# Which engine makes the low parts of the input pieces: GpSimd in place of VectorE for 171 of 243

## The chip, the cores and the metric

One NeuronCore of one Trainium2 chip runs the kernel. The metric is the device time of one execution in microseconds (us), smaller is better. Engines are named as in the profile: PE is TensorE, DVE is VectorE, ACT is ScalarE, POOL is GpSimd, SP is SyncE, which here only starts DMAs.

## The reference

Two attentions in a row for each of 8 batches and 8 heads (576 positions, head size 64, 32 packed queries), then two feed-forward layers on the 4608 tokens. All is float32; names are shortened here.

```python
def sm_attn(qq, kk, vv):
    s = scale * np.matmul(qq, kk.transpose(0, 1, 3, 2))
    s = s - np.max(s, axis=-1, keepdims=True)
    a = np.exp(s)
    a = a / (np.sum(a, axis=-1, keepdims=True) + 1e-09)
    return np.matmul(a, vv)
p_packed = sm_attn(p, k, v)
out = sm_attn(q, p_packed, p_packed)
...
h = x @ w_in                       # 512 -> 2048
g = np.maximum(h, 0.0) + alpha * np.minimum(h, 0.0)
y = g @ w_out                      # 2048 -> 512
...
g = y @ w_gate                     # 512 -> 1536
silu = g * (1.0 / (1.0 + np.exp(-g)))
val = y @ w_val
out = silu * val @ w_out2
```

## The kernel before

Every product is made from split operands. A float32 operand x is kept as a high part, x rounded to the type that TensorE multiplies fast (fp32r), and a low part, x minus the high part. `product` (L778 to L780) then issues three matmuls: high by high, low by high, high by low. The high part of an operand is a copy on ScalarE (L1119), the low part a subtraction on VectorE (`subtract`, L1441).

The inputs come in 243 pieces, each up to 128 x 576: 28 of keys ("k"), 35 of values ("v"), 28 of queries ("q"), 64 of w_in ("w"), 16 of w_out ("o"), and 72 for the second layer: 36 of its weights ("g") and 36 sums of them ("s"). SP loads a piece into a ring of four raw buffers (`load`, L605), once the low part of the piece four before it is made, since that frees the buffer. ScalarE makes the high part and VectorE the low part, both in `split`, into a second ring of four (`piece_`, tile name `piece`; w_out has its own place, tile name `w`). A slot of that ring is free once TensorE has used the piece, or, for "g" and "s", once a DMA that GpSimd starts has written it to DRAM (`w_scratch`, L760 and L762, `d_scratch`, L757). The semaphore `piece_high` counts high parts, `piece_split` low parts.

Each engine runs its own program in its own order. One list, `PLAN`, sets all of them. It has 256 slots, one for each of 16 chunks of 288 tokens by 16 tiles of w_in's columns. In a slot TensorE makes one tile of h (6 matmuls, names `h<-attn,mixed`), and adds the tile of two slots before to y (12 matmuls, `acc<-g,w`, L986 and L990). Between them ScalarE takes the negative part of h (L1276), VectorE combines it with alpha into gF (L1633), ScalarE makes g's high part (L1119), VectorE its low part (L1441, `g<-floats,g`). Each of these goes some slots ahead of its use. The attention of the following batches, the products with w_in that go ahead (`mix`, tiles `side` and `mixed`), the pieces ("split" entries, one to three slots before their use) and the keeping of the second layer's weights ("keep" entries) are put into the slots as further entries. Attention on VectorE is a chain: L1483 (maximum), L1578 (transposes), L1584, L1586 (subtract maximum), L1591 to L1595, L1601 (normalise), L1605 (transpose).

A piece's low part is waited for in five places: by SP for the raw ring, by TensorE (`piece_ready`), by GpSimd for a "keep", by the sums of second-layer weights on VectorE, and by ScalarE before the buffer of these sums is used again. GpSimd's own program has a few memsets, `clear` entries (a memset of packF), the keeps and the stores of y (L767).

After the slots the second layer runs from the kept weights in five runs; no input piece is made there.

Of the kernel before, what the change touches and what calls it, by code (L numbers as in the profile page):

```python
# [284 lines left out]

PIECES = [e[1] for e in PLAN if e[0] == "split"]
PIECE_NO = {p: n for n, p in enumerate(PIECES)}
RAWS = [p for p in PIECES if p[0] != "s"]
RAW_NO = {p: n for n, p in enumerate(RAWS)}
AHEAD = RAW_NO["g", EARLY_KEEPS - 1, 0]  # L290
# [28 lines left out]
def build(nc, kT, vS, qT, pT, w_in, w_out, alpha, w_gate, w_val, w_down, out):  # L319
# [3 lines left out]
    with ExitStack() as ctx:  # L323
# [43 lines left out]
        def f(at, n):  # L367
            return F[:, at:at + n]
# [107 lines left out]
        ident_zeroed, ident_ready = sem("ident_zeroed"), sem("ident_ready")  # L476
        both_zeroed, both0_zeroed, packF_zeroed = sem("both_zeroed"), sem("both0_zeroed"), sem("packF_zeroed")
        nalpha_ready = sem("nalpha_ready")
        piece_high, piece_split, piece_left = sem("piece_high"), sem("piece_split"), sem("piece_left")
        p_high, p_split = sem("p_high"), sem("p_split")  # L480
        scores1_done, max1_ready, exp1_done, rec_ready, den1_step = (
            sem("scores1_done"), sem("max1_ready"), sem("exp1_done"), sem("rec_ready"), sem("den1_step"))
# [78 lines left out]
            return (f(4224, 1024) if j < EARLY_KEEPS else late_sums[:, :])  # L561


        def unsplit(p):

            return weight_sums(p[1])[:, 512 * p[2]:512 * p[2] + 512] if p[0] == "s" else raw(p)
# [17 lines left out]
        def _(sp):  # L584
            once = Once(sp)

            def load(p):
                if RAW_NO[p] >= RING:
                    once.wait_ge(piece_split, PIECE_NO[RAWS[RAW_NO[p] - RING]] + 1)
                dst = raw(p)  # L590
                if p[0] == "k":
                    src = kT[p[1], p[2], :, :]
                elif p[0] == "q":
                    dst = dst.rearrange("p (i n) -> p i n", i=2)
                    src = qT[p[1], 2 * p[3]:2 * p[3] + 2, :, p[2] * CH:(p[2] + 1) * CH].rearrange("i p n -> p i n")
                elif p[0] == "v":
                    dst = dst[rows(p[2]), :]
                    src = vS[p[1], p[2] * P:min((p[2] + 1) * P, SEQ), :]
                elif p[0] == "w":
                    src = w_in[p[3] * P:(p[3] + 1) * P, p[2] * CW:(p[2] + 1) * CW]  # L600
                elif p[0] == "o":
                    src = w_out[p[1]]
                elif p[0] == "g":
                    src = (w_gate, w_val)[p[2]][p[1]] if p[1] < NT2 else w_down[2 * (p[1] - NT2) + p[2]]
                sp.dma_start(dst, src).then_inc(raw_landed[raw_slot(p)], 16)  # L605
# [29 lines left out]
            def load_y(r, ks=range(KD)):  # L635
                if r:
                    once.wait_ge(block_step, steps_to(r - 1, T_ORDER[-1]))
                else:
                    once.wait_ge(attn_split, NCH)
                    once.wait_ge(attnF_ready, NCH - 1)  # L640
                    once.wait_ge(piece_split, PIECE_NO["s", EARLY_KEEPS - 1, 1] + 1)
                once.wait_ge(y_stored, 16 * min(NCH, -(-(START_OF[r] + 2 * HALF[r]) // CH)))
                for k in ks:
                    sp.dma_start(yraw[:, k, :, 0:HALF[r]],
                                 yT[k, :, START_OF[r]:START_OF[r] + 2 * HALF[r]].rearrange("p (c n) -> p c n", c=2)
                                 ).then_inc(y_landed, 16)
# [86 lines left out]
        @block.gpsimd  # L733
        def _(pool):
            once = Once(pool)
            pool.dma_start(alphas, alpha).then_inc(alpha_landed, 16)
            nc.gpsimd.memset(ident, 0.0).then_inc(ident_zeroed, 1)
            once.wait_ge(ident_zeroed, 1)
# [4 lines left out]
            once.wait_ge(t1_done, 2)  # L743
            nc.gpsimd.memset(f(4224, 512), 0.0).then_inc(both0_zeroed, 1)
            for e in PLAN:
                if e[0] == "clear":
                    if e[1] == 1:
                        once.wait_ge(pT_done, 2)
                    else:
                        once.wait_ge(packT_done, e[1] - 1)  # L750
                    nc.gpsimd.memset(f(7104, 512), 0.0).then_inc(packF_zeroed, 1)
                elif e[0] == "keep":
                    p = pieces_of(e)[0]
                    once.wait_ge(piece_split, PIECE_NO[p] + 1)
                    if e[1] >= NT2:
                        for s in range(1 if e[2] == 0 else 2):
                            pool.dma_start(dS[e[1] - NT2, e[2], s], piece(p)[:, :, 256 * s:256 * s + 256].bitcast(F32)  # L757
                                           ).then_inc(kept[e[2]], 16)
                    elif e[2] == 1:
                        pool.dma_start(wS[e[1], :, 1, :, 256:512], piece(p)[:, :, 256:512].bitcast(F32)).then_inc(kept[e[2]], 16)  # L760
                    else:
                        pool.dma_start(wS[e[1], :, e[2], :, :], piece(p).bitcast(F32)).then_inc(kept[e[2]], 16)  # L762
                elif e[0] == "ycopy":
                    c = e[1]
                    once.wait_ge(y_copied_act, 2 * c + 2)
                    once.wait_ge(y_copied_dve, 2 * c + 2)
                    pool.dma_start(yT[:, :, c * CH:(c + 1) * CH].rearrange("m p n -> p m n"), ystage  # L767
                                   ).then_inc(y_stored, 16)
# [5 lines left out]
        def _(pe):  # L774
# [20 lines left out]
                once.wait_ge(mix_split, mixes_before(e))  # L795

            def piece_ready(p):
                once.wait_ge(piece_split, PIECE_NO[p] + 1)

            def scores1_0(half):  # L800
                once.wait_ge(p0_ready, 1)
# [313 lines left out]
        def _(act):  # L1115
# [87 lines left out]
            def exp1(e):  # L1203
                _, b, half = e
                once.wait_ge(max1_ready, NTH[e] + 1)
                if b == 1:
                    once.wait_ge(mix_done, 2 * KD)
                    once.wait_ge(rec1_ready, 2)
                else:
                    once.wait_ge(turned, ST * (b - 1))  # L1210
                    once.wait_ge(rec_ready, 2 * (b - 1))
                sums = before(e, "sums") // 2
                if sums:
                    once.wait_ge(piece_split, PIECE_NO["s", sums - 1, 1] + 1)
                nc.scalar.activation(s1[:, half, :].rearrange("p (c n) -> p c n", c=2), scores,
                                     ACT.Exp, bias=nmax1[:, half:half + 1], accum_out=sum1[:, half:half + 1]
                                     ).then_inc(exp1_done, 1)
# [129 lines left out]
            def copy_lead(r):  # L1347

                once.wait_ge(tile_done, NTILES * r + TILE_NO["B11", PAIRS - 1] + 1)
                if r == 0:  # L1350
                    once.wait_ge(y_stored, 16 * NCH)
                    once.wait_ge(piece_split, len(PIECES))
                once.wait_ge(out_stored[11], 16 * r)
                copy(lead[:, :, 0:HALF[r]], acc[:, 0:2, 0:HALF[r]]).then_inc(lead_copied, 1)

# [81 lines left out]
        def _(dve):  # L1437
# [2 lines left out]
            def subtract(dst, x, high):  # L1440
                return nc.vector.tensor_tensor(dst, x, high.bitcast(F32), ALU.subtract)  # L1441

            def split(p):
                n = PIECE_NO[p]
                k, c = piece_rows(p), piece_columns(p)
                once.wait_ge(piece_high, n + 1)
                subtract(piece(p)[k, 1, c], unsplit(p)[k, c], piece(p)[k, 0, c]).then_inc(piece_split, 1)

            def sums(e):

# [7 lines left out]
                if half == 0:  # L1458
# [1 line left out]
                    if j >= EARLY_KEEPS:  # L1460
                        once.wait_ge(packed_done, B - 1)
                    if j:
                        once.wait_ge(piece_split, PIECE_NO["s", j - 1, 1] + 1)
                    for p in (g_no, v_no):
                        once.wait_ge(raw_landed[raw_slot(p)], landed(p))
                    nc.vector.tensor_tensor(s1_, a21, a22, ALU.add).then_inc(sums_step, 1)
# [302 lines left out]
            for e in PLAN:  # L1769
# [15 lines left out]
                    attn_0(e[1])  # L1785
                elif e[0] == "alpha":
                    alpha_1()
                elif e[0] == "split":
                    split(e[1])
                elif e[0] == "split_p":  # L1790
                    split_p(e[1])
                elif e[0] == "max1":
# [117 lines left out]
```

## Time and profile before

| | |
|---|---|
| median of three runs | 1597.93 us (1597.17 to 1599.99) |
| the profiled execution | 1597.42 us, of which the span is 1595.2 us |
| PE busy | 98% |
| DVE busy | 72% |
| ACT busy | 46% |
| POOL busy | 5% |

The span is the stretch from the first to the last instruction that the profiler saw; all times of rows count from its start. A row of a timeline is one instruction, or several of one kind in a run; in brackets stands how long the engine was idle before it and which engine's instruction ended that. The first layer fills the span to about 800 us, the second the rest. Matmuls of 288 columns follow each other at about 0.13 us and are shown with their latency of 0.29 us, so that small gaps between them can't be seen as idle time.

### The profile page before, as it was taken

The numbers are of one execution on the slowest core, as the hardware profiler recorded it, in microseconds if no ns is written. First come the engines' busy times: TensorE is split into PE (matmuls) and PEld (weight loads), VectorE is DVE, ScalarE is ACT, GpSimd is POOL, SyncE is SP. The second block draws the span as 40 slices with busy tenths as digits, with TensorE's granted clock in tenths as the row PEclk, the third lists the DMA queues.
The fourth block names the chain that finished last, engine by engine and source line by source line (L and its number), as shares of the span: only waits on it lengthen the run. The fifth ranks groups of instructions, "written<-read, shape, count | busy, mean of one in ns | idle before, by whom it ended". The sixth has DMA issues, their size and how long they took to land.

```text
span 1595.2 us, 24866 instructions
## 1 busy us (share of the span) xinstructions
PE 1562.7 (98%) x9330; PEld 1436.2 (90%) x9330; DVE 1148.5 (72%) x2010; ACT 728.5 (46%) x1475; POOL 76.3 (5%) x123
## 2 busy tenths in 40 slices
PE   8999999999999999999999999999999999999999
PEld 5899988989999999999988888888888889999998
DVE  5777679868698687987865577556765685667666
ACT  4565568555685656745532144223412252233223
POOL 0000000100001000014300000000000000000000
PEclk9999999999999999999999999999999999999999
DMA  7343225523345233338665665766667667877856
GB/s 269 111 126 115 79 73 161 166 87 120 115 123 178 65 131 121 98 147 293 213 219 192 238 212 178 245 235 217 192 213 237 215 200 248 300 271 238 290 203 218
DMA packets 132502, 293.15 MB, mean 184 GB/s; under 512 B 13456, under 2 KB 41120, under 8 KB 132384
## 3 DMA queue, kind: packets, MB, share of 16 engines
q1 hardware_dynamic: 120544, 249.08, 49.0%
q0 software_dynamic: 11840, 42.48, 7.0%
q8 instruction: 75, 1.23, 0.3%
q14 instruction: 43, 0.35, 0.1%
HBM read 239.61 MB, written 51.90 MB: 183 GB/s over the span
## 4 chain that ended last, share of the span: by engine, by line
PE 80%; DVE 13%; ACT 3%; issue 2%; DMA 1%; ACTq 0%; DVEq 0%
PE acc L986 9%; PE side L778 9%; PE side L779 9%; PE side L780 9%; PE h L778 8%; PE h L780 8%; PE h L779 8%; PE acc L990 5%; PE acc L778 5%; PE acc L780 4%; PE acc L779 4%; DVE piece L1441 3%; DVE mixed L1441 2%; DVE floats L1633 2%; DVE g L1441 1%
## 5 line engine op out<-in xcount | busy, mean ns | idle before, releaser
L986 PE MATMUL acc<-g,w 128*128 128x288 f32 x1792 | 272.4, 294 | 0.0
L986 PEld LDWEIGHTS acc<-g,w 128*128 128x128 f32 x1792 | 249.0, 188 | 0.0
L1119 ACT ACTIVATE g<-floats 128x288 fp32r<-128x288 f32 x256 | 113.8, 444 | 223.3 <-DVE floats L1633 152.5
L1441 DVE TENSOR_TENSOR g<-floats,g 128x288 fp32r<-128x288 f32 x256 | 115.2, 450 | 68.0 <-ACT g L1119 66.5
L1323 ACT ACTIVATE rows_b<-side 128x512 f32<-128x512 f32 (+1 forms) x60 | 33.4, 557 | 285.6 <-PE side L780 285.6
L1441 DVE TENSOR_TENSOR piece<-floats,piece 128x512 fp32r<-128x512 f32 (+3 forms) x217 | 143.5, 682 | 25.2 <-ACT piece L1119 22.5
L778 PE MATMUL h<-attn,mixed 128*128 128x288 f32 x512 | 157.8, 308 | 3.5 <-DVE floats L1633 2.1
L1633 DVE SCALAR_TENSOR_TENSOR floats<-floats,h 128x288 f32<-128x288 f32 x256 | 130.4, 509 | 39.9 <-ACT floats L1276 38.3
L990 PE MATMUL acc<-g,w 128*128 128x288 f32 x896 | 156.2, 296 | 0.2 <-DVE g L1441 0.2
L780 PE MATMUL h<-attn,mixed 128*128 128x288 f32 x512 | 151.3, 295 | 0.0
L779 PE MATMUL h<-attn,mixed 128*128 128x288 f32 x512 | 151.2, 295 | 0.0
L990 PEld LDWEIGHTS acc<-g,w 128*128 128x128 f32 x896 | 131.2, 188 | 0.5 <-DVE g L1441 0.5
L1119 ACT ACTIVATE piece<-floats 128x512 fp32r<-128x512 f32 (+3 forms) x217 | 128.2, 616 | 3.5 <-PE side L780 2.1
L1276 ACT ACTIVATE floats<-h 128x288 f32<-128x288 f32 x256 | 102.7, 401 | 39.5 <-PE h L780 38.0
L778 PEld LDWEIGHTS h<-attn,mixed 128*128 128x128 f32 x512 | 96.3, 188 | 10.9 <-DVE floats L1633 3.1
L1329 ACT ACTIVATE rows_a<-rows_a 128x512 f32<-128x512 f32 (+1 forms) x60 | 35.4, 590 | 143.6 <-DVE rows_a L1696 143.6
L779 PEld LDWEIGHTS h<-attn,mixed 128*128 128x128 f32 x512 | 96.4, 188 | 3.3 <-issue 1.0
L780 PEld LDWEIGHTS h<-attn,mixed 128*128 128x128 f32 x512 | 96.3, 188 | 0.0
L1681 DVE TENSOR_TENSOR rows_b<-side,rows_a 128x512 f32<-128x512 f32 (+1 forms) x60 | 38.3, 638 | 71.6 <-PE side L780 71.3
L1671 DVE TENSOR_TENSOR rows_a<-side,rows_a 128x512 f32<-128x512 f32 (+1 forms) x60 | 38.3, 638 | 64.2 <-PE side L780 64.2
L1119 ACT ACTIVATE tiles_b<-u_a 128x512 fp32r<-128x512 f32 (+3 forms) x80 | 61.7, 778 | 47.2 <-PE acc L780 24.6
L1441 DVE TENSOR_TENSOR mixed<-side,mixed 64x512 fp32r<-64x512 f32 (+1 forms) x112 | 76.9, 687 | 5.1 <-ACT mixed L1119 3.8
(284 smaller groups left out, 3810.5 us busy)
## 6 DMA issues: line engine op xcount, KB each, us to landing
ring<-w_scratch SPq DMA_DIRECT2D x90, 512.0 KB, 4.4
wring<-d_scratch SPq DMA_DIRECT2D x168, 256.0 KB, 2.9
ring_c<-w_scratch SPq DMA_DIRECT2D x60, 512.0 KB, 4.1
w_scratch<-piece POOLq DMA_DIRECT2D x36, 512.0 KB, 4.0
floats<-w_in SPq DMA_DIRECT2D x64, 256.0 KB, 3.2
ring_b<-w_scratch SPq DMA_DIRECT2D x30, 512.0 KB, 4.8
d_scratch<-piece POOLq DMA_DIRECT2D x42, 256.0 KB, 3.8
ring<-d_scratch SPq DMA_DIRECT2D x42, 256.0 KB, 3.0
```

Source lines behind the costliest of these rows:

```text
L778: pe.matmul(dst, w[0], x[0], start=start, stop=False, **kw)
L779: pe.matmul(dst, w[1], x[0], start=False, stop=False, **kw)
L780: return pe.matmul(dst, w[0], x[1], start=False, stop=stop, **kw)
L986: pe.matmul(acc[:, m, 0:CH], w2[:, j, x, m * P:(m + 1) * P], g[:, s % 2, 0, :], start=False, stop=False)
L990: mm = pe.matmul(acc[:, m, 0:CH], w2[:, j, 0, m * P:(m + 1) * P], g[:, s % 2, 1, :], start=False, stop=False)
L1119: return nc.scalar.activation(dst, src, ACT.Copy, **kw)
L1276: nc.scalar.activation(gF[:, s % 2, :], hb[s % 2][:, 0:CH], ACT.Relu, scale=-1.0).then_inc(neg_done, 1)
L1329: nc.scalar.activation(first_two[:, 0:h], first_two[:, 0:h], ACT.Silu).then_inc(silu2_ready, 1)
L1441: return nc.vector.tensor_tensor(dst, x, high.bitcast(F32), ALU.subtract)
L1633: nc.vector.scalar_tensor_tensor(out=gF[:, s % 2, :], in0=gF[:, s % 2, :], scalar=alphas[:, j:j + 1], in1=hb[s % 2][:, 0:CH], op0=ALU.mult ...
L1671: nc.vector.tensor_tensor(first_two[:, 0:h], set_banks[1][:, 0:h], first_term[:, 0:h], ALU.add).then_inc(two_ready, 1)
L1681: nc.vector.tensor_tensor(first_three[:, 0:h], set_banks[1][:, 0:h], first_term[:, 0:h], ALU.add).then_inc(three_ready, 1)
```

## The change

Low parts of "k", "v", "q", "w" and "o" pieces, 171 of them, are made by GpSimd (`input_low`, `BY_POOL`), at the place of the "split" entry in GpSimd's program. The 72 of "g" and "s" stay on VectorE (`weight_low`, `BY_DVE`). GpSimd has a semaphore of its own, `input_split`; `low_of` tells each waiting engine which semaphore and value a piece has. High parts stay on ScalarE, and `PLAN` is the same. The memset of a `clear` waits for the low parts that stand ahead of it, and each low part for the one before it.

```diff
+BY_POOL = [p for p in PIECES if p[0] in "kvqwo"]
+BY_DVE = [p for p in PIECES if p[0] in "gs"]
...
+        def low_of(p):
+
+            return (input_split, BY_POOL.index(p) + 1) if p in BY_POOL else (piece_split, BY_DVE.index(p) + 1)
...
+            def input_low(p):
+                k, c = piece_rows(p), piece_columns(p)
+                once.wait_ge(input_split, BY_POOL.index(p))
+                once.wait_ge(both0_zeroed, 1)
+                once.wait_ge(packF_zeroed, before(("split", p), "clear") + 1)
+                once.wait_ge(piece_high, PIECE_NO[p] + 1)
+                nc.gpsimd.tensor_tensor(piece(p)[k, 1, c], unsplit(p)[k, c], piece(p)[k, 0, c].bitcast(F32), ALU.subtract
+                                        ).then_inc(input_split, 1)
...
             for e in PLAN:
-                if e[0] == "clear":
+                if e[0] == "split" and e[1] in BY_POOL:
+                    input_low(e[1])
+                elif e[0] == "clear":
...
+                    once.wait_ge(input_split, sum(p in BY_POOL for p in PIECES[:before(e, "split")]))
...
-            def split(p):
-                n = PIECE_NO[p]
-                k, c = piece_rows(p), piece_columns(p)
-                once.wait_ge(piece_high, n + 1)
-                subtract(piece(p)[k, 1, c], unsplit(p)[k, c], piece(p)[k, 0, c]).then_inc(piece_split, 1)
+            def weight_low(p):
+                c = piece_columns(p)
+                once.wait_ge(piece_high, PIECE_NO[p] + 1)
+                subtract(piece(p)[:, 1, c], unsplit(p)[:, c], piece(p)[:, 0, c]).then_inc(piece_split, 1)
```

Three places of the instruction order follow. The lines of the changed kernel are some 20 higher: L1441 is L1461 there, L1601 is L1620, L1633 is L1652.

The first is VectorE between the end of an attention chain and the next slots, at 497 to 502 us of the trace. `piece` of 576 columns is a query. Before:

```order
L1441 TENSOR_TENSOR g<-floats,g 128x288
L1441 TENSOR_TENSOR piece<-floats,piece 128x576
L1633 SCALAR_TENSOR_TENSOR floats<-floats,h 128x288
L1601 TENSOR_TENSOR floats<-floats 128x576
L1605 STREAM_TRANSPOSE floats<-floats 128x576
L1441 TENSOR_TENSOR g<-floats,g 128x288
L1441 TENSOR_TENSOR piece<-floats,piece 128x576
```

After:

```order
L1461 TENSOR_TENSOR g<-floats,g 128x288
L1652 SCALAR_TENSOR_TENSOR floats<-floats,h 128x288
L1620 TENSOR_TENSOR floats<-floats 128x576
L1624 STREAM_TRANSPOSE floats<-floats 128x576
L1461 TENSOR_TENSOR g<-floats,g 128x288
L1652 SCALAR_TENSOR_TENSOR floats<-floats,h 128x288
```

The two queries' low parts are gone from the row; all else keeps its order.

The second is GpSimd from 457 to 491 us, the end of the w_in pieces of batch 4 and the fifth set of second-layer weights. L762 and L760 before (L782 and L780 after) are keeps. Before:

```order
37 L767 DMA y_scratch<-floats 128x4x288 [waits y_copied_dve,y_copied_act]
38 L762 DMA w_scratch<-piece 128x1024 [waits piece_split]
39 L760 DMA w_scratch<-piece 128x2x256 [waits piece_split]
```

After:

```order
94 L787 DMA y_scratch<-floats 128x4x288 [waits y_copied_dve,y_copied_act]
95 L750 TENSOR_TENSOR piece<-floats,piece 128x512 [waits piece_high,input_split] x5
96 L750 TENSOR_TENSOR piece<-floats,piece 128x576 [waits piece_high,input_split] x2
97 L782 DMA w_scratch<-piece 128x1024 [waits piece_split]
98 L780 DMA w_scratch<-piece 128x2x256 [waits piece_split]
```

The keeps now stand behind two queries' low parts, whose high parts ScalarE makes later than the kept piece.

The third is VectorE at 566 to 572 us, a pair of keys that TensorE uses at once (`x2`), and pieces of the second layer around it. Before:

```order
L1578 STREAM_TRANSPOSE floats<-side 128x288 x2
L1441 TENSOR_TENSOR g<-floats,g 128x288
L1441 TENSOR_TENSOR piece<-floats,piece 128x576 x2
L1441 TENSOR_TENSOR piece<-floats,piece 128x512
L1633 SCALAR_TENSOR_TENSOR floats<-floats,h 128x288
```

After:

```order
L1597 STREAM_TRANSPOSE floats<-side 128x288 x2
L1461 TENSOR_TENSOR g<-floats,g 128x288
L1461 TENSOR_TENSOR piece<-floats,piece 128x512
L1652 SCALAR_TENSOR_TENSOR floats<-floats,h 128x288
```

The pair stands on GpSimd instead, between the keeps of the two 512-column pieces around it.

## Rows read from the trace of the kernel before

**Rows 1.** The page, busy time and share of the span of each engine.

```profile
PE 1562.7 (98%) x9330; PEld 1436.2 (90%) x9330; DVE 1148.5 (72%) x2010; ACT 728.5 (46%) x1475; POOL 76.3 (5%) x123
```

**Rows 2.** Table by stretch; columns: stretch, length, busy time by engine, clock, DMA.

```profile
30.00:700.00 670.00, 649.00 (x4640) 623.32 (x4639) 530.56 (x1057) 415.53 (x941) 36.63 (x59) 1.00 0.37 118
```

**Rows 3.** Groups by shape, VectorE: line, names, shapes, count, busy us, mean ns, idle before.

```profile
L1441 DVE TENSOR_TENSOR g<-floats,g 128x288 fp32r<-128x288 f32 x256 | 115.2, 450 | 68.0 <-ACT g L1119 66.5
L1441 DVE TENSOR_TENSOR piece<-floats,piece 128x512 fp32r<-128x512 f32 x136 | 91.8, 687 | 15.9 <-ACT piece L1119 13.9
...
L1441 DVE TENSOR_TENSOR piece<-floats,piece 128x576 fp32r<-128x576 f32 x56 | 40.2, 753 | 7.7 <-ACT piece L1119 7.3
...
L1441 DVE TENSOR_TENSOR w<-floats,w 128x512 fp32r<-128x512 f32 x16 | 11.0, 687 | 2.3 <-ACT w L1119 2.1
```

**Rows 4.** Groups by shape, GpSimd.

```profile
L751 POOL MEMSET floats<- 128x512 f32 x7 | 3.8, 542 | 6.0 <-PE h L830 6.0
...
L739 POOL TENSOR_SCALAR_AFFINE_SELECT floats<-floats 128x128 f32<-128x128 f32 x1 | 0.3, 282 | 0.2 <-POOL floats L737 0.2
...
L1904 POOL MEMSET const-float32-0.0<- 128x1 f32 x1 | 0.1, 99 | 0.2 <-issue 0.2
```

**Rows 5.** Timeline of PE, matmuls that waited: start, length, instruction, idle before.

```profile
76.93 0.39 PE L778 MATMUL side<-piece,pp 128*128 128x256 f32 x1 [1.41 <-DVE pp L1441]
...
158.91 0.39 PE L778 MATMUL side<-piece,pp 128*128 128x256 f32 x1 [0.68 <-DVE pp L1441]
...
209.40 0.38 PE L778 MATMUL side<-piece,pp 128*128 128x256 f32 x1 [0.69 <-DVE pp L1441]
...
230.87 0.53 PE L778 MATMUL side<-piece,both 128*128 128x512 f32 x1 [1.17 <-DVE both L1441]
...
248.03 0.50 PE L778 MATMUL side<-piece,both 128*128 128x512 f32 x1 [1.37 <-DVE mixed L1441]
...
286.70 0.40 PE L778 MATMUL h<-attn,mixed 128*128 128x288 f32 x1 [0.48 <-DVE floats L1633]
...
304.98 0.37 PE L778 MATMUL acc<-g,w 128*128 128x288 f32 x1 [0.85 <-DVE g L1441]
...
377.55 0.37 PE L778 MATMUL side<-piece,pp 128*128 128x288 f32 x1 [0.77 <-issue]
...
501.07 0.37 PE L778 MATMUL acc<-g,w 128*128 128x288 f32 x1 [0.84 <-DVE g L1441]
```

**Rows 6.** Timelines of DVE and PE's weight loads around three places with keys.

```profile
325.14 1.43 DVE L1441 TENSOR_TENSOR piece<-floats,piece 128x576 fp32r<-128x576 f32 x2 [1.11 <-ACT piece L1119]
...
326.62 0.19 PEld L778 LDWEIGHTS side<-piece,pp 128*128 128x128 f32 x1 [0.17 <-DVE piece L1441]
...
385.44 0.76 DVE L1441 TENSOR_TENSOR piece<-floats,piece 128x576 fp32r<-128x576 f32 x1 [1.11 <-ACT piece L1119]
...
386.63 0.19 PEld L778 LDWEIGHTS side<-piece,pp 128*128 128x128 f32 x1
...
569.42 2.03 DVE L1441 TENSOR_TENSOR piece<-floats,piece 128x576 fp32r<-128x576 f32 x3
...
570.90 0.19 PEld L778 LDWEIGHTS side<-piece,pp 128*128 128x128 f32 x1 [0.17 <-DVE piece L1441]
```

**Rows 7.** Timeline of DVE ahead of the wait at 501.07.

```profile
497.94 0.75 DVE L1441 TENSOR_TENSOR piece<-floats,piece 128x576 fp32r<-128x576 f32 x1
...
499.02 0.75 DVE L1601 TENSOR_TENSOR floats<-floats 128x576 f32<-128x576 f32 x1
```

**Rows 8.** Timelines of POOL and ACT, and the page's DMA issues (count, KB, us to landing).

```profile
474.97 0.53 POOL L762 DMA_DIRECT2D w_scratch<-piece  x1 [16.43 <-DVE piece L1441]
...
478.15 1.24 ACT L1119 ACTIVATE piece<-floats 128x576 fp32r<-128x576 f32 x2
...
485.43 0.61 ACT L1119 ACTIVATE piece<-floats 128x512 fp32r<-128x512 f32 x1
...
w_scratch<-piece POOLq DMA_DIRECT2D x36, 512.0 KB, 4.0
```

More of the change, by code:

```diff
@@ L478, in build @@
         nalpha_ready = sem("nalpha_ready")
-        piece_high, piece_split, piece_left = sem("piece_high"), sem("piece_split"), sem("piece_left")
+        piece_high, piece_left = sem("piece_high"), sem("piece_left")
+        piece_split, input_split = sem("piece_split"), sem("input_split")
         p_high, p_split = sem("p_high"), sem("p_split")
@@ L588, in load @@
                 if RAW_NO[p] >= RING:
-                    once.wait_ge(piece_split, PIECE_NO[RAWS[RAW_NO[p] - RING]] + 1)
+                    once.wait_ge(*low_of(RAWS[RAW_NO[p] - RING]))
                 dst = raw(p)
@@ L640, in load_y @@
                     once.wait_ge(attnF_ready, NCH - 1)
-                    once.wait_ge(piece_split, PIECE_NO["s", EARLY_KEEPS - 1, 1] + 1)
+                    once.wait_ge(*low_of(("s", EARLY_KEEPS - 1, 1)))
                 once.wait_ge(y_stored, 16 * min(NCH, -(-(START_OF[r] + 2 * HALF[r]) // CH)))
@@ L753, in _ @@
                     p = pieces_of(e)[0]
-                    once.wait_ge(piece_split, PIECE_NO[p] + 1)
+                    once.wait_ge(*low_of(p))
                     if e[1] >= NT2:
@@ L797, in piece_ready @@
             def piece_ready(p):
-                once.wait_ge(piece_split, PIECE_NO[p] + 1)
+                once.wait_ge(*low_of(p))
             def scores1_0(half):
@@ L1213, in exp1 @@
                 if sums:
-                    once.wait_ge(piece_split, PIECE_NO["s", sums - 1, 1] + 1)
+                    once.wait_ge(*low_of(("s", sums - 1, 1)))
                 nc.scalar.activation(s1[:, half, :].rearrange("p (c n) -> p c n", c=2), scores,
@@ L1351, in copy_lead @@
                     once.wait_ge(y_stored, 16 * NCH)
-                    once.wait_ge(piece_split, len(PIECES))
+                    once.wait_ge(piece_split, len(BY_DVE))
                 once.wait_ge(out_stored[11], 16 * r)
@@ L1462, in sums @@
                     if j:
-                        once.wait_ge(piece_split, PIECE_NO["s", j - 1, 1] + 1)
+                        once.wait_ge(*low_of(("s", j - 1, 1)))
                     for p in (g_no, v_no):
@@ L1787, in _ @@
                     alpha_1()
-                elif e[0] == "split":
-                    split(e[1])
+                elif e[0] == "split" and e[1] in BY_DVE:
+                    weight_low(e[1])
                 elif e[0] == "split_p":
```

## Prediction

> **What bounds the kernel now.** I read the page's busy shares first. TensorE is busy 98% of the span [rows 1], at a granted clock of 1.00 in the stretch that matters [rows 2], so a change elsewhere can only give back TensorE's idle time or add to it. Then the table by stretch: the moved subtractions stand between 30 and 700 us, and there TensorE is busy 649.0 of 670 us. So at most 21.0 us can be given back, while VectorE is busy 530.6 us and GpSimd 36.6 us [rows 2]. VectorE is the fuller of the two, but an average says little. What counts is which wait ends last in front of a matmul. The timeline of TensorE names it: nine of its larger waits in the stretch end on VectorE, or on a queue behind it, with a low part of an input piece shortly ahead in VectorE's row [rows 5]. And a few matmuls start the moment a low part of a key is made [rows 6]. These two lists are the two sides of the sum.
>
> **What is removed.** 171 of 243 low parts leave VectorE: 64 of w_in, 35 of values, 28 of keys, 28 of queries, 16 of w_out. 99 pieces of 512 columns at 687 ns are 68.0 us, 56 of 576 columns at 753 ns are 42.2 us, 16 of w_out at 687 ns are 11.0 us: 121.2 us in all [rows 3]. Nearly all of it lay beside matmuls. What was on the path is the part in front of TensorE's waits. At 497.94 a query's low part runs 0.75 us on VectorE; behind it come L1633, L1601, L1605 and the low part of g, and a matmul has waited 0.84 us for the last of these at 501.07 [rows 5, 7]. The order's first place shows the query's step gone from between them. In the same way I credit each wait with the moved low parts directly ahead of it, never more than the wait itself: 0.69 at 76.93, 0.68 at 158.91, 0.69 at 209.40, 0.69 at 230.87, 0.69 at 248.03, 0.48 at 286.70, 0.75 at 304.98, 0.77 at 377.55 (two keys ahead), 0.75 at 501.07. The sum is 6.2 us [rows 5]. That is the upper end. The lower end is zero: what is late next is the link of the chain that VectorE does not shorten (TensorE's turn, ScalarE's copy), and the subtractions that leave may cost VectorE something beside GpSimd (below). Waits whose VectorE row had been idle, or had only pieces of the second layer ahead, get no credit. Between the ends I take the middle, 3.1 us, since neither end has a row that is nearer.
>
> **What is added.** 171 subtractions on GpSimd. Its trace shows no instruction with two inputs, so the price is bounded. Below: the memset of 128x512, which only writes, took 542 ns, and TENSOR_SCALAR_AFFINE_SELECT, which reads one input, took 282 ns for 128 columns, against 99 ns for one column: 1.44 ns a column, which makes 0.84 us for 512 columns and 0.93 us for 576. Above: the same with the second input read after the first, 1.58 us and 1.76 us [rows 4]. A subtraction has two inputs, so it should lie over the one-input line; I take the middle, 1.2 us for 512 and 1.35 us for 576. The Trainium skill (GPSIMD Engine Reference, section 3.1) has 4497 ns for a tensor_tensor of 2048 columns. By that page an estimate would be 1.1 and 1.25 us, and the sum below would be about 0.6 us smaller. No run here shows it. In all it is some 205 us of GpSimd's 670, so throughput holds.
>
> A low part now comes 0.5 to 0.6 us later by itself, and the second of a pair 1.2 us later, since both queue on one slower engine. That costs nothing where the matmul comes several us later, as it does for most pieces; the cover is the lead that the plan gives. It costs where there is no lead. The second key of a pair is at 326.62: VectorE began the pair at 325.14, and the weights were loaded 0.05 us after its end [rows 6]. GpSimd starts about 0.17 us later than VectorE did (L739 there waited 0.2 us for a semaphore of its own engine [rows 4]; VectorE follows ScalarE at once), and then makes 2 x 1.35 us: 325.14 + 0.17 + 2.70 + 0.05 = 328.06, so 1.44 us later than 326.62. The pair at 569.42 with its matmul at 570.90 gives 1.43 us, and a third pair, at 579, repeats the pattern: 4.3 us. The single key at 385.44 gives 385.44 + 0.17 + 1.35 + 0.05 = 387.01 against 386.63, 0.4 us [rows 6]. Sum 4.7 us. With the low price (0.93 us, no later start) it is 3 x 0.4 = 1.2 us; with the high one (1.76 us) 3 x 2.3 + 0.8 = 7.6 us. The pieces of w_in with as little lead cost nothing: on VectorE they stood behind low parts of mixed and g, which GpSimd does not have.
>
> **What is moved past what.** GpSimd also issues the DMAs that keep the second layer's weights and store y. A DMA that stands behind a low part now waits for that piece's high part. At the order's second place the DMA of the first piece of a set, issued at 474.97, comes behind both queries [rows 8]. ScalarE makes both high parts from 478.15 on in 1.24 us, the first by about 478.8, so the DMA goes at about 478.8 + 0.2 + 2.7 = 481.7. With 4.0 us to landing that is 485.7, and ScalarE wants the slot at 485.43 [rows 8]: 0.3 us, hidden by the lead of its copies. Where landing takes longer it is the third rival. SP's loads of the input wait for the low part too, and go 0.5 to 1.2 us later; I cost them at nothing, since ScalarE's copies of pieces hardly waited for a load, and name the sign of the contrary below. The w_out pieces and the clears of packF are covered by several us of lead. After 700 us the order is unchanged, so nothing moves there.
>
> **The sum.** 4.7 - 3.1 = +1.6 us on a profiled execution of 1597.42 us (span 1595.2 and 2.2 around it), which stands 0.5 us under the median of the runs, 1597.93. I add it to the median: 1599.5.
>
> **The rivals.**
> First, faster. A low part takes about 0.93 us and VectorE gets all of its time back: +1.2 - 6.2, and the small waits among the 21.0 us give another 1: -6.0, so 1591.9. For it: VectorE is busy 79% of the stretch. Against it: GpSimd's one-input row already gives 0.93, and several of the listed waits are chains from a matmul over ScalarE back to TensorE.
>
> Second, slower, by one mechanism: a GpSimd subtraction and a VectorE instruction with both inputs in SBUF hold each other up. The trace of before cannot show it, since GpSimd there only writes beside VectorE. If one waits for the other's end, VectorE's low part of g (0.45 us, 256 times [rows 3]) or L1601 (0.75 us, [rows 7]) stands up to 1.35 us behind a GpSimd step where its own low part took 0.75. Nothing is then given back, each pair of keys is parted by one VectorE instruction of 0.45 us (3 x 0.45 = 1.4 us), and slots with little lead lose about 1 us: 4.7 + 1.4 + 1.0 = +7.1, so 1605.0. It decides as soon as both engines cannot read at once. The Trainium skill (SBUF — State Buffer, "Who interferes with whom") states just this rule: a VectorE instruction with two SBUF inputs and a GpSimd instruction that reads SBUF exclude each other for a whole instruction. By that rule the time is 1605.0; L1633 and the subtractions from PSUM, with one SBUF input, would be free of it.
>
> Third, late refills: DMAs that keep weights land late, ScalarE's next copy into the slot waits, and with it the high part of g. Four places at 1 us each beyond the forecast: 1603. Against it: other keeps have 7 us or more from issue to reuse.
>
> That the change does not do what it says is ruled out by the order: 171 subtractions stand on GpSimd.
>
> **How the numbers follow.** Forecast 1599.5, chance 0.45, its own range 1596 to 1602. Faster rival 0.24, mutual hold-up 0.23, late refills 0.08. Leaving out about 0.1 at either end gives 1591.5 to 1606. A measurement can tell about 0.2%, 3.2 us, from no change. Faster by that (under 1594.7): 0.20, all from the first rival. Slower (over 1601.1): 0.07 of the forecast, 0.21 of the hold-up, 0.05 of the refills, 0.33. Within: 0.47.
>
> **What would show it.** Right: GpSimd's new group of subtractions has a mean near 1.2 and 1.35 us; VectorE's group of g keeps 450 ns and L1601 0.75 us; the second keys near 327, 571 and 580 us follow waits of over 1 us for GpSimd; the wait at 501.07 is down to about 0.1. Wrong: VectorE's two-input instructions grow or start late with nothing ahead of them while L1633 keeps its length (the hold-up); the new group has a mean under 1 us (faster); ScalarE's copies wait for w_scratch or a load (refills).

## The result and the profile after

The changed kernel takes 1614.55 us (median, 1613.89 to 1616.02). Measured beside it, the kernel before takes 1598.41 us. The ratio is 1.0102, 95% interval 1.0084 to 1.0119: slower by about 16 us, outside the predicted range of 1591.5 to 1606. The profiled execution took 1615.05 us, with a span of 1612.9 us against 1595.2.

The page, busy time and share of the span of each engine; and, from its chain that ended last, the shares by engine:

```profile
PE 1567.3 (97%) x9330; PEld 1439.7 (89%) x9330; DVE 1107.0 (69%) x1839; ACT 731.0 (45%) x1475; POOL 310.6 (19%) x294
...
PE 78%; DVE 15%; ACT 3%; issue 2%; DMA 1%; POOL 1%; SPq 0%; ACTq 0%; DVEq 0%; POOLq 0%
```

Beside [rows 1], VectorE lost 171 instructions, which the prediction put at 121.2 us of work, and its busy time fell by 41.5 us only. TensorE does the same 9330 matmuls, yet is busy 4.6 us longer and idle 13.1 us longer; together these are the 17.7 us by which the span grew. The next views say why. First VectorE and GpSimd by shape (line, names, shapes, count, busy us, mean ns, idle before):

```profile
L1461 DVE TENSOR_TENSOR g<-floats,g 128x288 fp32r<-128x288 f32 x256 | 166.0, 648 | 78.6 <-ACT g L1139 77.1
L1652 DVE SCALAR_TENSOR_TENSOR floats<-floats,h 128x288 f32<-128x288 f32 x256 | 130.3, 509 | 105.0 <-ACT floats L1296 103.7
L1461 DVE TENSOR_TENSOR mixed<-side,mixed 64x512 fp32r<-64x512 f32 x96 | 66.0, 687 | 7.5 <-ACT mixed L1139 6.3
L1461 DVE TENSOR_TENSOR piece<-floats,piece 128x512 fp32r<-128x512 f32 x44 | 34.3, 781 | 8.1 <-ACT piece L1139 7.2
...
L1620 DVE TENSOR_TENSOR floats<-floats 128x576 f32<-128x576 f32 x15 | 15.9, 1061 | 0.0
...
L1605 DVE TENSOR_TENSOR floats<-floats 128x576 f32<-128x576 f32 x15 | 13.9, 928 | 0.5
```

```profile
L750 POOL TENSOR_TENSOR piece<-floats,piece 128x512 fp32r<-128x512 f32 x92 | 121.1, 1316 | 158.1 <-ACT piece L1139 156.0
L750 POOL TENSOR_TENSOR piece<-floats,piece 128x576 fp32r<-128x576 f32 x56 | 83.0, 1482 | 102.2 <-ACT piece L1139 100.2
...
L750 POOL TENSOR_TENSOR w<-floats,w 128x512 fp32r<-128x512 f32 x16 | 21.3, 1329 | 28.3 <-ACT w L1139 27.9
```

The low part of g, untouched by the change, went from a mean of 450 ns [rows 3] to 648 ns. The pieces of 512 columns that stayed went from 687 to 781 ns, L1620 (L1601 before) from 0.75 us [rows 7] to 1061 ns. All of these read two inputs from SBUF. L1652 and the low part of `mixed` read one operand from PSUM (`h`, `side`); they stand at 509 and 687 ns, and in the zero-filled kernels below, where GpSimd reads nothing, L1652 again has 511 ns. I sorted the 256 low parts of g by whether a GpSimd subtraction was under way: 183 without one have a mean of 0.452 us, 73 with one 1.141 us, the longest 2.06 us. Of the low parts of g that began while a subtraction ran (68), 60 ended 0.31 to 0.33 us after its end and none later than 0.42 us after it, however much of it was still to run. GpSimd is held too: its subtractions of 512 columns took 1.41 us in the mean where a VectorE TENSOR_TENSOR with both inputs in SBUF was under way at their start (24), and 1.29 us where none stood beside them (42); with 576 columns 1.60 us (18) and 1.43 us (15).

What such a meeting looks like stands at the very place for which the prediction expected a wait to shrink to 0.1 us. The timeline of all engines at 509.75 to 514.4 us (start, length, engine, instruction, idle before):

```profile
509.87 1.57 POOL L750 TENSOR_TENSOR piece<-floats,piece 128x576 fp32r<-128x576 f32 x1 [4.16 <-ACT piece L1139]
510.06 0.50 DVE L1652 SCALAR_TENSOR_TENSOR floats<-floats,h 128x288 f32<-128x288 f32 x1
510.48 1.56 DVE L1620 TENSOR_TENSOR floats<-floats 128x576 f32<-128x576 f32 x1
...
512.08 0.78 DVE L1624 STREAM_TRANSPOSE floats<-floats 128x576 f32<-128x576 f32 x1
512.14 1.41 POOL L750 TENSOR_TENSOR piece<-floats,piece 128x576 fp32r<-128x576 f32 x1
512.78 1.09 DVE L1461 TENSOR_TENSOR g<-floats,g 128x288 fp32r<-128x288 f32 x1
...
514.02 0.37 PE L798 MATMUL acc<-g,w 128*128 128x288 f32 x1 [1.79 <-DVE g L1461]
```

L1652 (one SBUF input) keeps its 0.50 us beside the GpSimd step. L1620 starts beside it and ends 0.60 us after its end at 511.44; the low part of g ends at 513.87, 0.32 us after GpSimd's end at 513.55. Here the query's low part, 0.75 us, is gone from VectorE, but L1620 takes 0.81 us more and g 0.68 us more (its length at 500.51 was 0.41 us before), and the matmul, which had waited 0.84 us before [rows 5], now waits 1.79 us.

TensorE's groups of matmuls that wait, by name; the idle time before them is the last column (before the change, in the same order: 3.5, 0.2, 9.0, 2.4 and 3.3 us):

```profile
L798 PE MATMUL h<-attn,mixed 128*128 128x288 f32 x512 | 157.7, 308 | 4.3 <-DVE floats L1652 2.9 <-DVE attn L1461 1.2
L1010 PE MATMUL acc<-g,w 128*128 128x288 f32 x896 | 157.1, 297 | 1.1 <-DVE g L1461 1.1
L798 PE MATMUL side<-piece,pp 128*128 128x288 f32 (+2 forms) x126 | 38.8, 308 | 14.1 <-POOL piece L750 5.9 <-DVE pp L1461 3.6 <-issue 3.0
L798 PE MATMUL acc<-g,w 128*128 128x288 f32 x128 | 38.4, 300 | 7.0 <-DVE g L1461 5.0 <-DVE floats L1667 2.0
L798 PE MATMUL side<-piece,both 128*128 128x512 f32 x64 | 25.9, 405 | 6.2 <-DVE mixed L1461 4.9 <-DVE both L1461 1.0 <-POOL piece L750 0.3
```

They add up to 14.3 us more (all other groups together wait 1.2 us less), in two kinds: matmuls that wait for GpSimd's low part of a piece, and matmuls that wait for VectorE, although VectorE has fewer instructions than before: for its low parts of g and of `mixed`, and for L1667, a copy out of PSUM (2.0 of the 7.0 us). The low part of `mixed` keeps its length, so it comes late by what stands ahead of it. At the longest wait, which ends at 249.79, that is a low part of g of 1.41 us, where before the change it took 0.46 us; from its start to that of the low parts of `mixed` it is 4.05 us instead of 3.71, although a piece's 0.69 us between them is gone.

The third part is the clock. Table by stretch, TensorE alone (stretch, length, busy, granted clock, DMA share, GB/s); before the change the clock is 1.00 in the stretch [rows 2]:

```profile
249.00:251.00 2.00, 1.21 (x7) 1.00 0.39 112
251.00:253.00 2.00, 2.00 (x12) 0.56 0.47 88
253.00:255.00 2.00, 2.00 (x10) 0.58 0.90 331
255.00:257.00 2.00, 2.00 (x16) 1.00 0.65 106
333.00:335.00 2.00, 1.24 (x6) 0.54 0.55 146
335.00:337.00 2.00, 2.00 (x10) 0.50 0.38 120
337.00:339.00 2.00, 2.00 (x11) 0.50 0.00 0
339.00:341.00 2.00, 2.00 (x13) 0.75 0.03 8
341.00:343.00 2.00, 2.00 (x17) 1.00 0.02 4
```

In two places TensorE runs at 1.2 GHz instead of 2.4. The first follows a wait of 2.10 us for the low part of `mixed` that ends at 249.79, the second the waits for the first pair of keys (1.92 us, then 0.76 us). The missing clock shares, 0.44 and 0.42 of 2 us and 0.46, 0.50, 0.50 and 0.25 of 2 us, sum to 5.1 us. That is at most what the half clock costs, since TensorE was also idle in part of it, and it is near the 4.6 us by which its busy time grew. The split is rough: short gaps between matmuls count as busy, and zero_lows below, which never had the half clock, is busy 3.0 us less than the kernel before.

Which wait is followed by the half clock isn't shown. In keys_stay (below) TensorE waits 2.08 us for the same low part of `mixed`, until 249.84, and the clock stays at 1.00. Of the other profiled executions quarters has 17.1 us at half clock, against 10.2 us here; zero_late, keys_zero, only_w, only_q and only_vo have one stretch of 3.4 us each, and the rest none before the end of the span.

### The profile page after: what moved, and what is told of

Read it like the earlier page. It is cut to its first block, busy times and chain, and to the rows that moved or that the text cites. A ratio compares the mean times of both kernels' runs of the same rounds, so it can differ in the third digit from the quotient of the medians.

```text
span 1612.9 us, 25044 instructions
## 1 busy us (share of the span) xinstructions
PE 1567.3 (97%) x9330; PEld 1439.7 (89%) x9330; DVE 1107.0 (69%) x1839; ACT 731.0 (45%) x1475; POOL 310.6 (19%) x294
## 4 chain that ended last, share of the span: by engine, by line
PE 78%; DVE 15%; ACT 3%; issue 2%; DMA 1%; POOL 1%; SPq 0%; ACTq 0%; DVEq 0%; POOLq 0%
PE side L798 9%; PE acc L1006 9%; PE side L800 8%; PE side L799 8%; PE h L798 8%; PE h L800 8%; PE h L799 8%; PE acc L798 4%; PE acc L800 4%; PE acc L799 4%; PE acc L1010 4%; DVE g L1461 3%; DVE mixed L1461 2%; DVE floats L1652 2%; DVE piece L1461 1%
## 5 line engine op out<-in xcount | busy, mean ns | idle before, releaser
L750 POOL TENSOR_TENSOR piece<-floats,piece 128x512 fp32r<-128x512 f32 (+1 forms) x155 | 213.2, 1375 | 275.3 <-ACT piece L1139 271.1
L1461 DVE TENSOR_TENSOR g<-floats,g 128x288 fp32r<-128x288 f32 x256 | 166.0, 648 | 78.6 <-ACT g L1139 77.1
L1652 DVE SCALAR_TENSOR_TENSOR floats<-floats,h 128x288 f32<-128x288 f32 x256 | 130.3, 509 | 105.0 <-ACT floats L1296 103.7
L1010 PE MATMUL acc<-g,w 128*128 128x288 f32 x896 | 157.1, 297 | 1.1 <-DVE g L1461 1.1
L1010 PEld LDWEIGHTS acc<-g,w 128*128 128x128 f32 x896 | 131.9, 189 | 2.0 <-DVE g L1461 2.0
L1461 DVE TENSOR_TENSOR mixed<-side,mixed 64x512 fp32r<-64x512 f32 (+1 forms) x112 | 76.9, 687 | 8.2 <-ACT mixed L1139 7.0
```

Of the source, the lines that this page charges most:

```text
L750: nc.gpsimd.tensor_tensor(piece(p)[k, 1, c], unsplit(p)[k, c], piece(p)[k, 0, c].bitcast(F32), ALU.subtract).then_inc(input_split, 1)
L1010: mm = pe.matmul(acc[:, m, 0:CH], w2[:, j, 0, m * P:(m + 1) * P], g[:, s % 2, 1, :], start=False, stop=False)
L1652: nc.vector.scalar_tensor_tensor(out=gF[:, s % 2, :], in0=gF[:, s % 2, :], scalar=alphas[:, j:j + 1], in1=hb[s % 2][:, 0:CH], op0=ALU.mult ...
```

## The experiments

All ran beside the kernel before, in three rounds. "Low parts" are those that the change moves.

| kernel | median, us | ratio, 95% interval |
|---|---|---|
| zero_lows: zeros by two memsets on GpSimd | 1590.41 | 0.9951 [0.9937, 0.9966] |
| short_lows: nearly all cut to 32 columns | 1588.54 | 0.9939 [0.9924, 0.9954] |
| zero_late: zeros by three memsets | 1597.88 | 1.0000 [0.9990, 1.0009] |
| keys_stay: all but the keys on GpSimd | 1607.48 | 1.0064 [1.0044, 1.0084] |
| only_keys: keys (28) on GpSimd | 1606.12 | 1.0050 [1.0033, 1.0067] |
| keys_zero: keys on GpSimd, as zeros | 1599.28 | 1.0005 [0.9995, 1.0014] |
| only_w: w_in (64) on GpSimd | 1601.89 | 1.0028 [1.0017, 1.0040] |
| only_q: queries (28) on GpSimd | 1599.48 | 1.0018 [1.0009, 1.0028] |
| only_vo: values and w_out (51) | 1598.21 | 1.0006 [0.9996, 1.0016] |
| quarters: four instructions a low part | 1614.07 | 1.0110 [1.0095, 1.0125] |

### GpSimd busy for as long, but reading nothing

The theory by now was the second rival of the prediction, the mutual hold-up. Against it stood that GpSimd's low parts are simply late. zero_lows keeps every semaphore and every place of the changed kernel and takes only the reads away:

```diff
-                nc.gpsimd.tensor_tensor(piece(p)[k, 1, c], unsplit(p)[k, c], piece(p)[k, 0, c].bitcast(F32), ALU.subtract
-                                        ).then_inc(input_split, 1)
+                once.wait_ge(piece_high, PIECE_NO[p] + 1)
+                nc.gpsimd.memset(piece(p)[k, 1, c].bitcast(F32), 0.0).then_inc(zero_step, 1)
+                once.wait_ge(zero_step, BY_POOL.index(p) + 1)
+                nc.gpsimd.memset(piece(p)[k, 1, c].bitcast(F32), 0.0).then_inc(input_split, 1)
```

> GpSimd fills the low part of its 171 pieces with zeros, twice with a wait between, in place of the subtraction (the low by high terms of these pieces drop out of the result). It keeps GpSimd's place, queue and about its length (2 x 0.54 us and a wait of 0.2 us, against 1.3 us alone), but reads nothing. Hold-up of reads: VectorE's two-input groups are back at 0.45 and 0.75 us, the time is 1597 to 1602 us. Late low parts as the cause: it stays at 1610 us or more.

Groups by shape of zero_lows, VectorE and GpSimd:

```profile
L1464 DVE TENSOR_TENSOR g<-floats,g 128x288 fp32r<-128x288 f32 x256 | 115.4, 451 | 81.3 <-ACT g L1142 79.8
L1464 DVE TENSOR_TENSOR piece<-floats,piece 128x512 fp32r<-128x512 f32 x44 | 30.2, 688 | 8.1 <-ACT piece L1142 7.2
...
L1623 DVE TENSOR_TENSOR floats<-floats 128x576 f32<-128x576 f32 x15 | 11.3, 752 | 0.0
```

```profile
L752 POOL MEMSET piece<- 128x512 f32 x92 | 48.5, 527 | 164.2 <-ACT piece L1142 162.2 <-POOL floats L774 0.4
L754 POOL MEMSET piece<- 128x512 f32 x92 | 48.4, 526 | 5.3
L752 POOL MEMSET piece<- 128x576 f32 x56 | 32.5, 580 | 108.3 <-ACT piece L1142 106.9
```

The page of zero_lows, busy time:

```profile
PE 1559.7 (98%) x9330; PEld 1434.6 (90%) x9330; DVE 1045.8 (66%) x1839; ACT 730.9 (46%) x1475; POOL 261.1 (16%) x465
```

1590.41 us: 7.5 us under the kernel before, 24 us under the changed one (ratios 0.9951 and 1.0102). It is also under the 1597 to 1602 us that the expectation gave the hold-up, and far from the 1610 us of lateness. A low part here takes 1.11 us (512 columns) or 1.22 us (576) on GpSimd, 0.21 and 0.26 us less than the subtraction. VectorE's lengths are back at those of before, and it is busy 61.2 us less than in the changed kernel; g alone is 50.6 us of that. Against the kernel before it is busy 102.7 us less, and not 121.2: instructions that follow each other at once overlap in the record (two of 753 ns are a run of 1.43 us in [rows 6]). So the change takes 102.7 us of busy time off VectorE and puts 61.2 us back, which leaves the 41.5 us. VectorE's relief is real and worth what the faster rival gave it; what the change loses beyond lateness is in the reading.

short_lows shortens the subtraction itself: all but the first eight low parts and those of w_out cover 32 columns (274 ns each), so most low parts are left stale.

```diff
+                c = c if p[0] == "o" or RINGED.index(p) < 8 else slice(0, 32)
```

> As the changed kernel, but GpSimd subtracts only 32 columns of a piece, except for w_out and the first eight others (the rest of these low parts is stale). Hold-up of reads: each one is short, VectorE has its 121 us back, 1590 to 1597 us; the gap to 1598.4 is what the relief is worth. Late low parts: the same. If the two semaphores or the order on GpSimd cost the time, it stays near 1610 us.

1588.54 us, just under the expected 1590 to 1597, with g at 477 ns. This is the gain if the low parts cost GpSimd hardly anything, only 1.9 us beyond zero_lows. The low parts are not zeros here, so the gain of zero_lows does not come from TensorE multiplying zeros.

### How much is lateness

zero_late adds a third memset to each low part, in the same way as the second. A low part of zeros then takes 1.69 us (512 columns) or 1.86 us (576), longer than the changed kernel's means of 1.32 and 1.48 us, with no read.

> All 171 moved low parts are filled with zeros by three memsets each in a row on GpSimd, about 1.75 us for 512 columns and 1.85 us for 576, so each is later than the subtraction of the changed kernel (1.32 and 1.48 us), yet nothing of it reads SBUF. The computed result is not the reference's. If the loss is the hold-up alone, this stays near the kernel with two memsets, 1590 to 1596 us, as only the pairs of keys are late by another 1.3 us each. If lateness of the low parts is a real part of the loss, it goes above 1598 us.

1597.88 us, 7.8 us over zero_lows (ratios 1.0000 and 0.9951) by the ratios. It fell between the two expected ranges, 1590 to 1596 for the hold-up alone and over 1598 for lateness as a real part. So lateness has a price: 0.6 us more on each low part takes the whole relief away. TensorE's groups of matmuls with idle before them, in zero_lows and then in zero_late:

```profile
L801 PE MATMUL acc<-g,w 128*128 128x288 f32 x128 | 38.4, 300 | 1.3 <-DVE g L1464 1.1
L801 PE MATMUL side<-piece,pp 128*128 128x288 f32 (+2 forms) x126 | 38.0, 301 | 6.7 <-POOL piece L754 2.8 <-issue 2.1 <-DVE floats L1600 1.5
```

```profile
L803 PE MATMUL acc<-g,w 128*128 128x288 f32 x128 | 38.4, 300 | 1.3 <-DVE g L1466 1.2
L803 PE MATMUL side<-piece,pp 128*128 128x288 f32 (+2 forms) x126 | 38.1, 303 | 10.6 <-POOL piece L756 6.9 <-issue 2.1 <-DVE floats L1602 1.5
```

Lateness shows mainly where TensorE waits for GpSimd (6.9 us here, 2.8 in zero_lows, 5.9 in the changed kernel); the wait for g stays at 1.3 us, where the changed kernel has 7.0. With low parts that are later than the changed kernel's in the mean, zero_late is still 16 us faster than that (ratios 1.0000 and 1.0102). If later low parts can't make a kernel faster, which no run tests, this bounds what the hold-up costs with all that follows from it, the half clock included: at least 16 us, against zero_late, and at most 24 us, against zero_lows, whose low parts are a little early.

### Which pieces

Four kernels move the sets one at a time, or all but one, by one line:

```diff
-BY_POOL = [p for p in PIECES if p[0] in "kvqwo"]
-BY_DVE = [p for p in PIECES if p[0] in "gs"]
+BY_POOL = [p for p in PIECES if p[0] in "k"]
+BY_DVE = [p for p in PIECES if p[0] not in "k"]
```

("vqwo" in keys_stay, "w", "q" and "vo" in the others.)

> The 28 keys stay on VectorE, 143 low parts are made by GpSimd. Hold-up of reads: the waits at three pairs of keys go (about 5 us of the 16), but the others stay: 1608 to 1612 us. Late low parts as the cause: nearly all comes back, 1600 us or less.

> Only the 28 keys are made by GpSimd. Hold-up of reads: 1602 to 1606 us, the pairs cost 5 us. Late low parts as the cause: most of the 16 us is here, 1609 us or more.

> Only the 64 pieces of w_in are made by GpSimd. By the hold-up each low part costs where VectorE's row is full, so a share of the 16 us by their number (64 of 171, less the key pairs): 1600 to 1606 us. If relief counted for more than the hold-up here, 1594 to 1598.

> Only the 28 queries. They stand beside the attention chain (L1586, L1601 of before) in VectorE's fullest slots. Hold-up: 1600 to 1606 us, with L1620 held in the profile. By my prediction's relief (0.75 us at 304.98, 0.77 at 377.55 is keys, 0.75 at 501.07): 1595 to 1598.

> Only the 35 pieces of values and 16 of w_out, which TensorE uses 4 us or more after the high part. Few of VectorE's two-input instructions stand beside them: 1596 to 1602 us; a gain over 1597.9 only if relief is larger than the hold-up.

In us over before, by the ratios: keys 8.0, w_in 4.5, queries 2.9, values and w_out 1.0, together 16.4 against 16.3 for the whole change. The 28 keys are a sixth of the moved pieces and half of the loss. keys_stay, without the keys, is still 10.2 us slower than before by the ratio. Its executions spread with the clock: 1605.93 and 1606.00 us at a granted clock of 1.000, 1608.96 at 0.998 and 1613.19 at 0.996. So some 8 us of its loss need no half clock. Of the ranges expected for the hold-up, only_w and only_vo lie inside; keys_stay is 0.5 us under its own, only_keys 0.1 us over, and only_q 0.5 us under, above the 1595 to 1598 of the prediction's relief.

keys_zero has the keys alone on GpSimd, filled with zeros by two memsets, for the question whether the keys lose by being late, as the prediction had it, or by the hold-up.

> Only the 28 low parts of keys are on GpSimd, and they are filled with zeros by two memsets each (about 1.2 us), which read nothing; the other 215 low parts are VectorE's. The computed result is therefore not the reference's. If the 8.2 us that the keys cost on GpSimd are the hold-up of reading instructions, this kernel is at or under the kernel before, 1593 to 1598 us, with VectorE's group of g at 450 ns. If they are the lateness of the second key of each pair (the 4.7 us of the prediction), the lateness is the same here as there, and it stays at 1601 to 1605 us.

1599.28 us, ratio 1.0005 against 1.0050 with real subtractions, between the expected ranges of 1593 to 1598 (hold-up) and 1601 to 1605 (lateness), and nearer the first. About 7 us of the keys' 8 go when two memsets stand in for the subtraction. Matmuls that waited for GpSimd at two key pairs, timeline of TensorE in keys_zero and then in only_keys:

```profile
325.22 0.37 PE L801 MATMUL side<-piece,pp 128*128 128x288 f32 x1 [1.50 <-POOL piece L754]
...
326.40 0.61 PE L801 MATMUL side<-piece,pp 128*128 128x288 f32 x1 [0.55 <-POOL piece L754]
...
571.04 0.37 PE L801 MATMUL side<-piece,pp 128*128 128x288 f32 x1 [0.89 <-POOL piece L754]
...
572.23 0.40 PE L801 MATMUL side<-piece,pp 128*128 128x288 f32 x1 [0.55 <-POOL piece L754]
```

```profile
326.31 0.37 PE L798 MATMUL side<-piece,pp 128*128 128x288 f32 x1 [1.92 <-POOL piece L750]
...
327.70 0.40 PE L798 MATMUL side<-piece,pp 128*128 128x288 f32 x1 [0.77 <-POOL piece L750]
...
573.74 0.37 PE L798 MATMUL side<-piece,pp 128*128 128x288 f32 x1 [1.12 <-POOL piece L750]
...
575.47 0.40 PE L798 MATMUL side<-piece,pp 128*128 128x288 f32 x1 [1.09 <-POOL piece L750]
...
585.48 0.40 PE L798 MATMUL side<-piece,pp 128*128 128x288 f32 x1 [1.01 <-POOL piece L750]
```

The waits stand at the same places, and are longer by 0.2 to 0.5 us each with reads; the third pair, at 585.48, has none of this size in keys_zero. GpSimd at the three pairs in only_keys:

```profile
324.76 2.88 POOL L750 TENSOR_TENSOR piece<-floats,piece 128x576 fp32r<-128x576 f32 x2 [5.85 <-ACT piece L1139]
...
572.19 3.22 POOL L750 TENSOR_TENSOR piece<-floats,piece 128x576 fp32r<-128x576 f32 x2 [0.77 <-ACT piece L1139]
...
582.11 3.31 POOL L750 TENSOR_TENSOR piece<-floats,piece 128x576 fp32r<-128x576 f32 x2 [6.19 <-ACT piece L1139]
```

A pair of keys takes 2.49 us as four memsets (323.86 to 326.35 in keys_zero). As subtractions it takes 2.88 us at the first place, where no two-input instruction of VectorE is under way when one of them starts, and 3.22 and 3.31 us at the others, where one is (a piece's low part at 573.17, L1620 at 583.28). So what sets the two kernels apart is in part that a subtraction is plainly longer, some 0.4 us a pair, and in part that GpSimd itself is held up. No run parts the two, and for the keys lateness and hold-up stay mixed. Over all key and query matmuls (`side<-piece,pp`) the idle time is 13.7 us in only_keys and 10.3 in keys_zero, and at L1010, which waits for g, 1.1 us in only_keys and 0.0 in keys_zero. These 3.4 and 1.1 us are the 4.5 us by which the two profiled spans differ (1601.6 and 1597.1). The clock works the other way here: from 300 to 400 us it is 1.00 in only_keys and 0.98 in keys_zero. But the profiled execution of only_keys, 1603.76 us, is the fastest of its four; the others took 1605.95 to 1606.75 us at a clock of 0.996 to 0.998 over the run, so in them part of the 8 us is the half clock.

### Shorter instructions on GpSimd

If VectorE waits only for the GpSimd instruction under way, four short ones in place of one long should free it.

```diff
+                w = piece_size(p) // 4
+                for i in range(4):
+                    c = slice(w * i, w * i + w)
+                    ins = nc.gpsimd.tensor_tensor(piece(p)[k, 1, c], unsplit(p)[k, c], piece(p)[k, 0, c].bitcast(F32),
+                                                  ALU.subtract)
+                ins.then_inc(input_split, 1)
```

> As the changed kernel, but each of GpSimd's subtractions is cut into four of 128 or 144 columns, about 0.4 us each. If VectorE waits only for the instruction under way, its two-input instructions lose at most 0.4 us a time: the group of g falls from 648 to 520 ns or less, and the time to 1598 to 1606 us. If the four hold it together, it stays at 1612 us or more (each costs GpSimd a start of about 0.1 us too).

Groups by shape of quarters, VectorE, GpSimd and TensorE:

```profile
L1465 DVE TENSOR_TENSOR g<-floats,g 128x288 fp32r<-128x288 f32 x256 | 130.5, 510 | 77.6 <-ACT g L1143 76.0
```

```profile
L753 POOL TENSOR_TENSOR piece<-floats,piece 128x128 fp32r<-128x128 f32 x368 | 173.5, 502 | 109.6 <-ACT piece L1143 106.0
```

```profile
L802 PE MATMUL side<-piece,pp 128*128 128x288 f32 (+2 forms) x126 | 39.2, 311 | 17.1 <-POOL piece L753 11.4 <-issue 3.2 <-DVE floats L1601 1.5
L802 PE MATMUL acc<-g,w 128*128 128x288 f32 x128 | 38.5, 300 | 2.1 <-DVE g L1465 2.0
```

As expected, VectorE was freed: g has 510 ns instead of 648, and the matmuls that use it wait 2.1 us instead of 7.0. But four quarters cost 4 x 502 ns, 2.0 us a low part, and TensorE waits 11.4 us for GpSimd instead of 5.9. The clock is 0.995 over the run (0.997 in the changed kernel). 1614.07 us, where 1598 to 1606 had been expected for a freed VectorE: the loss was moved, not removed. No kernel of the set with full arithmetic beats the kernel before; moving values and w_out alone equals it.

## Why the prediction was wrong, point by point

**What bounds the kernel.** Right, and it held in every run: TensorE at 97 to 98%, and each change showed as its idle time or its clock. That at most 21.0 us could be won was right too; nothing said that 16 could not be lost.

**What is removed.** The credit was mis-sized. The full 6.2 us would have been nearer: zero_lows gains 7.5 us net of its own lateness, so the relief alone is more. The prediction halved it for want of a row, partly because of the hold-up, which is a separate cost and in the end outweighed it. Where nothing held VectorE up, in zero_lows, the waits for g did shrink (`acc<-g,w` from 2.4 to 1.3 us). The wait of 501.07, which was to fall to 0.1 us, is 0.31 us there and 1.79 us in the changed kernel.

**What is added.** The price on GpSimd was taken as 1.2 and 1.35 us, between 0.84 and 1.76. It came out at 1.32 and 1.48 us, inside the bounds; without VectorE beside it, some 1.29 us for 512 columns. In all 234 us of GpSimd more; the prediction had 205, though its own prices give 214 (115 at 1.2 us and 56 at 1.35). The middle between the bounds was a fair choice, and the estimate of 1.1 and 1.25 us, worked out from the Trainium skill (GPSIMD Engine Reference, section 3.1), was further off.

**Late keys.** The places were right: over 1 us of waiting for GpSimd at the pairs (1.92 us and then 0.76; 1.08 and 1.10 us at 584.59 and 586.32; 1.00 us at 596.31). The 4.7 us cannot be read apart from the keys' own relief; with zeros, in a pair that is 0.4 us or more shorter, the two together cost 0.8 us (interval -0.8 to 2.2). But the prediction priced lateness at four key places alone. zero_late shows that another 0.6 us on all low parts costs 7.8 us, so the cover that was claimed for "most pieces" was thinner than said: at 1.1 to 1.2 us it mostly holds, at 1.7 to 1.9 us it does not.

**What is moved past what.** Keeps land in 4.6 us instead of 4.0, and ScalarE's copies of pieces waited 1.5 us in all for a keep's DMA, against 0.7 before, one wait each. The third rival, four places at 1 us each, did not come.

**The sum.** The step that failed is the one that took VectorE's instructions at their old lengths. The sum had a term for the work that VectorE gives away and none for what the rest of its work costs beside GpSimd. That term measures 61 us of VectorE's busy time and 16 to 24 us at the end of the run, by zero_late and zero_lows, where the forecast was +1.6 us and the result +16.

**The second rival** was the right mechanism, with all its signs: g and L1601 grow, L1633 keeps its length. It had a chance of 0.23 and a price of 7.1 us. The chance was too low: two-input instructions of VectorE stand in nearly every slot, and the trace of before had no row against it. The Trainium skill (SBUF — State Buffer, "Who interferes with whom") states that a VectorE instruction with two SBUF inputs and a GpSimd instruction that reads SBUF exclude each other for a whole instruction; the traces agree in both halves (0.452 against 1.141 us for g, 451 ns beside memsets). The price was mis-sized in two terms. "Slots with little lead lose about 1 us" was a guess for what was the main cost: the waits for the low parts of g grew by 2.8 and 0.9 us and those for `mixed` by 3.5 us. And a half clock followed, up to 5 us, which no term had. The price "up to 1.35 us behind a GpSimd step" for one meeting was about right: g loses 0.69 us in the mean of 73 meetings, 1.6 us at most.

## What to carry to other kernels

Before moving elementwise work from VectorE to GpSimd, count the inputs: if GpSimd's instructions read SBUF and VectorE's have two SBUF inputs, each meeting serialises them, and the work that stays grows. Here 103 us of VectorE's busy time moved away and 61 us came back, in front of a TensorE that was 98% busy. A stand-in that occupies GpSimd about as long without reading (memsets) tells such a cost from plain lateness, and a second stand-in that is longer than the real work prices the lateness; one stand-in alone leaves the difference in length open, as with the keys. Splitting the GpSimd instruction in four shortened each hold-up but made the low part longer (2.0 us instead of 1.32), and gained nothing here; where its result isn't wanted soon it might, which no run shows.

## What the runs showed of the hardware

- A subtraction or multiplication on VectorE (TENSOR_TENSOR) with both inputs in SBUF that began during a GpSimd subtraction did not end before it: 60 of 68 low parts of g ended 0.31 to 0.33 us after it, L1620 in the case shown 0.60 us after it. For g 0.45 us became 1.14 us in the mean. GpSimd's subtraction of 512 columns grew from 1.29 to 1.41 us where it began during such an instruction. Instructions with one SBUF input kept 0.50 to 0.51 us beside it.
- GpSimd's subtraction took 274 ns for 32 columns, 502 ns for 128, 1316 ns for 512 and 1482 ns for 576.
- GpSimd's memsets of the same buffers, 526 to 580 ns each, left VectorE's lengths as they were (g 451 ns in zero_lows).
- After waits of TensorE of about 2 us its granted clock was 0.50 (1.2 GHz) for 3.4 and 6.8 us, in two places, at a cost of at most 5.1 us. It did not follow every such wait: in keys_stay TensorE waited 2.08 us until 249.84 and was busy only 25.84 of the 30 us from 240 to 270 (28.47 before the change), at a clock of 1.00. What decides is not settled here.
